# A two-layer MLP kernel: x times w_in by seven products on halves of a token tile, with weights streamed for every tile

## What is computed

```python
def _moe_ref(x, w_in, w_out, s, b):      # x (2304, 512), w_in (512, 2048), w_out (2048, 512)
    h = x @ w_in
    r = np.maximum(h, 0.0)
    g = s * (r * r) + b
    return g @ w_out

def _moe2_ref(x, w_in, w_out, alpha):
    h = x @ w_in
    g = np.maximum(h, 0.0) + alpha * np.minimum(h, 0.0)
    return g @ w_out

# reference: attention -> x; x = _moe_ref(x, ...); return _moe2_ref(x, ...)
```

## Time and profile before

| | us |
|---|---|
| median of 3 runs | 1132.96 (1132.89 to 1134.08) |
| the profiled execution, its own time | 1132.73 |
| its span in the trace | 1130.9 |
| TensorE busy | 1102.4 (97%) |
| VectorE busy | 524.1 (46%) |
| ScalarE busy | 518.0 (46%) |
| GpSimd busy | 263.9 (23%) |
| mean granted clock of TensorE | 0.998 |

### The profile page before, as it was taken

The page is one execution under the profiler, slowest core; times in us unless marked ns, Lnnn a source line. Parts: engine busy times, 40 slices in busy tenths (PEclk is TensorE's granted clock), DMA queues, the critical chain, the costliest instruction groups (busy, mean ns, idle before and its releaser), DMA issues.

```text
span 1130.9 us, 19159 instructions
## 1 busy us (share of the span) xinstructions
PE 1102.4 (97%) x5881; PEld 888.6 (79%) x5881; DVE 524.1 (46%) x1008; ACT 518.0 (46%) x925; POOL 263.9 (23%) x440
## 2 busy tenths in 40 slices
PE   6899999999999999999999999899999999999998
PEld 5677777777668888888888889788888888888887
DVE  6778888878833342242233236622332332232232
ACT  4677777777754432232232226633333333333343
POOL 2555565656554400000000007800000000000000
PEclk9999999999999999999999999999999999999999
DMA  6666565655311100000000004400000000000010
GB/s 154 149 165 145 135 150 129 151 131 128 92 34 52 47 19 0 0 0 0 0 0 0 0 0 131 131 1 1 27 11 0 0 37 0 0 37 0 0 39 19
DMA packets 100118, 59.75 MB, mean 53 GB/s; under 512 B 67040, under 2 KB 83440, under 8 KB 100080
## 3 DMA queue, kind: packets, MB, share of 16 engines
q1 hardware_dynamic: 100080, 59.28, 20.8%
HBM read 30.94 MB, written 4.72 MB: 32 GB/s over the span
## 4 chain that ended last, share of the span: by engine, by line
PE 89%; ACT 3%; POOL 3%; SPq 2%; issue 1%; DVE 1%; DMA 0%; ACTq 0%; DVEq 0%
PE psum L822 23%; PE psum L821 23%; PE psum L823 23%; PE psum L927 8%; PE psum L900 6%; PE psum L843 2%; ACT pt L566 2%; PE psum L845 2%; PE psum L829 2%; PE psum L897 1%; POOL wout_lo L471 1%; POOL win_lo L468 1%; SPq L366 1%; PE psum L908 1%; SPq L342 1%
## 5 line engine op out<-in xcount | busy, mean ns | idle before, releaser
L821 PE MATMUL psum<-x_hi,win_hi 128*128 128x512 f32 (+1 forms) x640 | 238.9, 373 | 1.4 <-DVE x_lo L752 1.4
L822 PE MATMUL psum<-x_lo,win_hi 128*128 128x512 f32 (+1 forms) x640 | 238.4, 373 | 0.0
L823 PE MATMUL psum<-x_hi,win_lo 128*128 128x512 f32 (+1 forms) x640 | 238.4, 372 | 0.0
L821 PEld LDWEIGHTS psum<-x_hi,win_hi 128*128 128x128 f32 x640 | 120.5, 188 | 25.2 <-DVE x_lo L752 2.5
L822 PEld LDWEIGHTS psum<-x_lo,win_hi 128*128 128x128 f32 x640 | 120.6, 188 | 23.0
L823 PEld LDWEIGHTS psum<-x_hi,win_lo 128*128 128x128 f32 x640 | 120.3, 188 | 23.2
L770 DVE SCALAR_TENSOR_TENSOR act_r<-act_n,nalpha,act_r 128x512 f32<-128x512 f32 (+1 forms) x80 | 55.8, 698 | 158.9 <-ACT act_r L624 158.6
L695 DVE TENSOR_REDUCE negm<-psum 128x1 f32<-128x576 f32 x144 | 108.0, 750 | 44.6 <-PE psum L845 41.5
L491 POOL TENSOR_SCALAR ex<-ex,none_in,rinv 128x576 f32<-128x576 f32 x144 | 118.8, 827 | 24.9 <-DVE rinv L714 23.2
L762 DVE SCALAR_TENSOR_TENSOR g_lo<-act_r,b_c,g_hi 128x512 fp32r<-128x512 f32 (+1 forms) x80 | 60.6, 758 | 134.3 <-ACT g_hi L616 134.3
L616 ACT ACTIVATE g_hi<-act_r,b_c 128x512 fp32r<-128x512 f32 (+1 forms) x80 | 54.6, 682 | 147.4 <-PE psum L823 124.8
(11 more groups left out here) (80 smaller groups left out, 1627.6 us busy)
## 6 DMA issues: line engine op xcount, KB each, us to landing
k_twice<-k_hi SPq DMA_DIRECT2D x64, 144.0 KB, 2.5
stage<-in_moe_w_out_dram SPq DMA_DIRECT2D x32, 256.0 KB, 2.7
k_low_half<-k_lo SPq DMA_DIRECT2D x32, 144.0 KB, 2.5
out_dram<-stage SPq DMA_DIRECT2D x18, 256.0 KB, 2.2
raw_q<-in_q_dram SPq DMA_DIRECT2D x32, 128.0 KB, 2.4
raw_k<-in_k_dram SPq DMA_DIRECT2D x32, 128.0 KB, 2.5
raw_v<-in_v_dram SPq DMA_DIRECT2D x32, 128.0 KB, 2.6
q_both<-q_hi SPq DMA_DIRECT2D x32, 128.0 KB, 2.3
```

What stands on the lines that cost most here:

```text
L821: nc.tensor.matmul(dst, lhs[0], rhs[0], start=first, stop=False)
L822: nc.tensor.matmul(dst, lhs[0], rhs[1], start=False, stop=False)
L823: return nc.tensor.matmul(dst, lhs[1], rhs[0], start=False, stop=final)
```

## The change

One pipeline of steps takes the place of the two layers' loops. A step is a pair of hidden chunks, j and j + 8 (`PJ` is 8), of one tile.

For a full tile w_in (two hidden chunks by four feature chunks) is taken as a 2 by 2 block matrix A, and x (four feature chunks by 512 tokens) as a 2 by 2 block matrix B of halves with two feature chunks and 256 tokens each. Instead of eight block products there are seven, in the scheme with 15 sums: four sums of w_in blocks (S1 to S4, `win_sum`), four of x blocks (T1 to T4, `x_sum`), and seven sums of products. One block product is 2 chunks by 3, so 6 matmuls of 256 columns, and a step has 42 of them where two chunks of before had 24 of 512. TensorE adds two products in PSUM where it can (`in_a` takes two, `in_c` and `in_d` two with a sum read between); the rest are `first_sum` on ACT (a copy of `in_a`) and `middle_sums` and `last_sums` on DVE (five additions of 256 columns, each of one PSUM and one SBUF operand). The rest tile of 256 tokens is computed with plain products.

TensorE's order in a step k is: `up_part1` (four products, 24 matmuls), `down` of step k-1 for its first hidden chunk (12 matmuls of 512), `up_part2` (three products, 18 matmuls, after `middle_sums` of step k), `down` of step k-1 for its second chunk.

Weights are no longer kept. Every step loads its 512 KB of w_in and 512 KB of w_out, for every tile anew, into two buffers each, and splits them: ACT casts 512, 256 and 1,024 columns of w_in and its sums and 1,024 of w_out, POOL makes the low parts of w_in and of one half of w_out (`w_low`, `wout_low`), DVE makes four weight sums (`w_sums`) and the low part of the other half. The x sums stand at j = 5 of the tile before, the casts and low parts of x at j = 7; ahead of a rest tile at j = 6. The finished tile is copied out of PSUM at j = 1 of the next (`acc_copy`).

The core of the diff:

```diff
+            def up_part1(layer, i, j):
+                par, k = j % 2, step_no(layer, i, j)
+                wait_alone(pe, r_ok, 2 * (k - 1))
+                pe.wait_ge(w_lo_ok, w_parts(layer, i, j) + FULL_W)
+                x_there(layer, i, j, 1)
+                product(in_a[par], par, A11, B11, True, False)
+                x_there(layer, i, j, 2)
+                product(in_d[par], par, S1, T1, False, True).then_inc(part1_a_done, 1)
+                x_there(layer, i, j, 3)
+                product(in_b[par], par, S2, T2, True, False)
+                product(in_c[par], par, S3, T3, False, True).then_inc(part1_done, 1)
+            def up_part2(layer, i, j):
+                par = j % 2
+                pe.wait_ge(mid_ok, full_no(layer, i, j) + 1)
+                x_there(layer, i, j, 4)
+                product(in_a[par], par, A12, B21, False, False)
+                x_there(layer, i, j, 5)
+                product(in_d[par], par, S4, B22, False, True).then_inc(part2_a_done, 1)
+                x_there(layer, i, j, 6)
+                product(in_c[par], par, A22, T4, False, True).then_inc(up_done, 1)
...
+            # VectorE, one step
+            def mlp_step(layer, i, j):
+                following = after(layer, i, j)
+                tile_after = after(layer, i, PJ - 1)
+                if j == 1 and tile_before(layer, i):
+                    acc_copy(*tile_before(layer, i))
+                if following and not is_rest(following[1]):
+                    w_sums(*following)
+                if not is_rest(i):
+                    middle_sums(layer, i, j)
+                wout_low(layer, i, j)
...
+                    if j == PJ - 3:
+                        x_sums(*tile_after[:2])
+                    if j == PJ - 1:
+                        x_low(*tile_after[:2], range(3))
+                if not is_rest(i):
+                    last_sums(layer, i, j)
+                for row in range(2):
+                    curve(layer, i, j, row)
+                for row in range(2):
+                    g_low(layer, i, j, row)
+                if j == PJ - 1 and not is_rest(i) and not is_rest(tile_after[1]):
+                    x_low(*tile_after[:2], range(3, FULL_X))
...
+            # GpSimd, one step
+            def mlp_step(layer, i, j):
+                following = after(layer, i, j)
+                if following:
+                    w_low(*following)
+                wout_low(layer, i, j)
...
+            # ScalarE, one step
+                if following:
+                    w_high(*following, range(2))
+                if not is_rest(i):
+                    first_sum(layer, i, j)
+                if following and not is_rest(following[1]):
+                    w_high(*following, [2])
+                wout_high(layer, i, j)
...
+                rectify(layer, i, j)
+                for row in range(2):
+                    g_high(layer, i, j, row)
```

More of the change, by code:

```diff
@@ new lines, in g_high @@
+            def g_high(layer, i, j, row):
+                par, k, n = j % 2, step_no(layer, i, j), width(i)
+                wait_alone(act, down_done, 2 * (k - 2) + row + 1)
+                act.wait_ge(t_ok, 2 * k + row + 1)
+                dst, src = g_hi[:, par, row, 0:n], act_r[:, par, row, 0:n]
+                if layer:
+                    nc.scalar.copy(dst, src).then_inc(g_hi_ok, 1)
+                else:
+                    nc.scalar.activation(dst, src, ACT.Identity, bias=b_c[:]).then_inc(g_hi_ok, 1)
@@ new lines, in acc_copy @@
+            def acc_copy(layer, i):
+                act.wait_ge(down_done, 2 * PJ * (layer * NT + i + 1))
+                if layer == 0:
+                    for c in range(CC):
+                        nc.scalar.copy(x_raw[:, c, bass.ds(i * TOK, width(i))], acc[c][:, 0:width(i)]).then_inc(acc_free, 1)
+                else:
+                    for sub in range(0, subs(i), 2):
+                        wait_alone(act, y_out[sub], DMA * i)
+                        nc.scalar.copy(y_sb[:, sub, :], acc[sub]).then_inc(y_ok[sub], 1)
@@ L965, in down1 @@
-            def down1(i, j, weight):
-                pe.wait_ge(g_ok, i * FC + j + 1)
-                wait(pe, w_ok, weight)
-                if j == 0:
-                    pe.wait_ge(acc_free, (i + 1) * DC)
-                for c in range(DC):
-                    lhs = [x[:, j, c * P:(c + 1) * P] for x in (wout_hi, wout_lo)]
-                    rhs = [x[:, j % 2, 0:width(i)] for x in (g_hi, g_lo)]
-                    mm = three(acc[c][:, 0:width(i)], lhs, rhs, j == 0, j == FC - 1)
-                mm.then_inc(down_done, 1)
@@ L1013 @@
+            mlp(pe, mlp_step)
+            for row in range(2):
+                down(1, FULL_TILES, PJ - 1, row)
 _INS = ["q", "k", "v", "tau", "moe_w_in", "moe_w_out", "moe_s", "moe_b", "moe2_w_in", "moe2_w_out", "moe2_alpha"]
```

693 lines of the change are left out of this document (403 added, 290 removed).

## The result

The changed kernel takes 1268.94 us (median; 1266.36 to 1271.02) where the kernel before takes 1132.93: 1.120 times, 95% interval 1.118 to 1.121. So it is 12.0% slower; the forecast was 9.7%, 1243 us, and the time lies inside the forecast's range of 1150 to 1290. The profiled execution took 1269.77 us, its span is 1268.0.

A forecast was written before the change was run, and what follows sets the result against it. DVE's path, with waits for POOL and ACT, was taken to bound full steps. 326.9 + 3 + 749 + 64 + 90 + 2 + 2 + 4 = 1241 us of span, so 1243 us, range 1150 to 1290.

The forecast's parts named there:

- TensorE's part: In full tiles, a step needs 10.44 us of matmuls, 0.64 less than before; 41 us over 64 steps.
- The engines' part: In full steps, DVE's path, shut out by POOL, sets 11.3 us in layer 1, 12.1 in layer 2: 749 us.
- the lock: In SBUF, DVE with two SBUF inputs and POOL exclude each other for a whole instruction; 2.6 us a step.
- the 0.20 us: At POOL's end, a shut-out DVE instruction starts 0.20 us before the rule's letter allows; the letter adds 38 us.
- Tile ends: At j = 5, 7 and 1, DVE's x sums, low parts and copies add in full: 64 us together.
- Rest tiles: In rest tiles, steps of 5.64 and 5.60 us, 90 us; POOL and DVE fit except x sums, 2 us.
- Start: Ahead of the MLPs, nine ACT casts add 4.97 us before the last products with v; MLPs start at 326.9.
- (a): In full steps and tile ends, the port costs half: layer 1 at 10.44, layer 2 at 11.2; 1154 us; chance 0.18.
- (b): In full steps, TensorE stays the bound at 10.44 us, tile ends cost 26 in all; 1124 us; chance 0.08.
- (c): At six tile ends, TensorE's clock falls after long waits, 9.5 us each, 57 in all: 1300 us; chance 0.10.
- (d): In TensorE's narrow matmuls, the weight load limits the pace at 0.19 us; excluded by starts 0.1175 apart, no chance given.

The follow-up runs named there:

- the split: POOL makes two low parts of 512 columns a full step, held until DVE reads PSUM, against DVE making all low parts, with later casts: 1162.77 us.
- the kernel with the other hand-over: DVE starts its sums after POOL's last normalisation, ACT makes three casts one position earlier, against the kernel with DVE's list reordered: 1149.80 us.
- undoing the hold: POOL's two waits on part1_done and part2_a_done removed, against the fastest: 1147.98 us.
- the fastest: ACT's u1 copy and w_out cast, DVE's 1,024-column low part and tile copy moved earlier at tile ends, against the kernel with the other hand-over: 1124.14 us.

## Why the prediction was right, and where its sizes were off

The path was the one forecast, and the sum was 27 us short: 2.8 at the start, 20.2 and 7.2 in the rest tiles, some 2 at the first step and the tail, less 5.0 in layer 2's full steps.

**TensorE's part: right in kind, 0.16 us a step short.** 10.44 us were summed, 10.60 is what a step takes once nothing else bounds it (POOL cut to one column, and all kernels after the split). The starts of its groups in such a stretch, with no wait between (timeline of PE, the kernel with the other hand-over):

```profile
911.68 0.28 PE L1153 MATMUL psum<-x_hi,w_hi 128*128 128x256 f32 x1
...
914.56 0.40 PE L1017 MATMUL psum<-wout_hi,g_hi 128*128 128x512 f32 x1
```

That is 2.88 us for 24 matmuls of 256 columns, 0.120 each and not 0.1175 as in the earlier trace rows; 42 × 0.0025 = 0.1 us of the difference; the rest is in the two groups of w_out. Seven products give 0.5 us a step against 11.08, some 31 us, not 41.

**The engines' part: right.** Steps of 11.33 and 12.12 us, at the very places where they were worked out; TensorE idle ahead of part 2, released by L902. Taking POOL's columns away removes the excess; undoing the hold brings 0.5 and 1.2 us a step back in a kernel with less than half of POOL's columns. The Trainium skill's rule ("SBUF — State Buffer", section "SBUF: two separate sides") has the lock; the 0.20 us that the forecast kept from the trace held again (`wout_lo` ends at 576.39; the rule's letter gives 576.53 there).

**Tile ends: right in sum.** The x sums cost +3.7 for 3.55, the last step +5.2 for 5.35, the copies +2.1 to 2.4 in layer 1 and +0.5 to 1.6 in layer 2 for 1.1. Against that, the last full tile is cheaper than counted: its last two steps make no or fewer weight sums for a rest tile (10.78 and 8.49 us for 12.1 in layer 2). I had left that out. That layer 1's full steps come to 392.94 for 392.9 is therefore in part luck: two errors of some 6 us cancel.

**Rest tiles: the term that was mis-sized.** "POOL's 3.9 us and DVE's 3.2 fit beside them, except for the x sums": 47 us were forecast for layer 1, 67.21 came. The step failed by its own rule: the lock was counted in full steps and forgotten here. DVE and POOL in a rest step:

```profile
745.61 2.56 POOL L528 TENSOR_TENSOR w_lo<-win_raw,w_hi 128x512 fp32r<-128x512 f32 x2 [4.40 <-ACT w_hi L605]
748.13 1.74 POOL L544 TENSOR_TENSOR wout_lo<-wout_raw,wout_hi 128x512 fp32r<-128x512 f32 x1
```

```profile
747.04 1.68 DVE L936 TENSOR_TENSOR wout_lo<-wout_raw,wout_hi 128x512 fp32r<-128x512 f32 x1 [1.50 <-ACT wout_hi L611]
748.64 1.78 DVE L865 TENSOR_TENSOR x_lo<-x_raw,x_hi 128x512 fp32r<-128x512 f32 x1
```

Both of DVE's stand ahead of the curve, and both are shut out, 1.0 and 1.1 us. Steps took 6.75 for 5.64, and those at the borders to full tiles 8.7 to 10.8, since a full tile's weights or `g` are made there. With POOL cut to one column this stretch takes 52.69 us, so some 14 of the 20 us are POOL's columns, and 6 are left at the borders. The last stretch of layer 2 is +7 for the forecast, and 5 of these go with POOL's columns (41.25 us for 46.62).

**Start: +2.8 for two reasons not in the sum.** The last products with v began 1.2 us later than summed (325.18 for 323.99) and took 1.5 us longer. ACT's casts cost 5 us, as counted. But DVE's early sums met POOL's last normalisations, for which the last copies of `pt` wait: two of them took 3.50 us together (0.83 each alone), and none took over 0.84 where the sums were held back. What this was worth by itself was not measured, since the casts moved in the same run. And the last products with v, after TensorE had waited 6.3 us, ran at the lower level for their first 3 us:

```profile
325.18 4.39 PE psum L1098 x20
```

against 2.91 in the earlier trace rows; the granted clock was 0.50 from 325.2 to 327 us, 0.54 to 328.3 and 1.00 behind that.

**Rivals.** (a) fell: DVE was shut out for 3.0 us a step by its records, and 2.6 were counted. (b) fell for this kernel; but what spoke for it, that "POOL and DVE need not meet if ACT feeds them at other moments", is what the last kernels use. That the fastest takes 1124.14 us, the very sum of (b), is in part luck: its steps are 10.60 us and not (b)'s 10.44, and those ahead of the rest tile are shorter than (b) had them. (c) came in part. The clock did fall at tile ends. TensorE had waited 1.9 us for `g_lo` (until 402.3) ahead of the first of these stretches, and 1.8 us for `g_lo` (until 428.8) and 3.75 for L902 (until 435.6) ahead of the second:

```profile
404.00:408.00 4.00, 3.58 (x13) 2.41 (x13) 3.14 (x7) 1.92 (x2) 1.71 (x3) 0.66 0.00 0
435.00:442.00 7.00, 6.37 (x26) 5.93 (x27) 5.03 (x8) 3.54 (x7) 4.09 (x2) 0.58 0.18 63
```

(stretch, busy PE, PEld, DVE, ACT, POOL, clock, DMA share, GB/s). The Trainium skill's rule that idle gaps bring the lower level back ("TensorE: Matmul & The Clock Gate", section "Why this matters for your kernels") agrees with these stretches. The 9.5 us a tile end were not paid: in layer 1 the last step and the two behind it (16.54 + 13.75 + 11.32 us) come within 1.3 us of the forecast without a fall (16.65 + 12.4 + 11.3). The likely reason, argued and not tested, is that a slower pace is taken out of TensorE's waits where it isn't the bound; at the start, where it was, it cost 1.5 us. (d) fell: the narrow matmuls start 0.120 us apart and not 0.19.

## What to carry to other kernels

When work is handed to GpSimd to relieve VectorE, look first at where VectorE's operands lie: beside instructions with both operands in SBUF, a part of GpSimd's time is added and not hidden (here 149 us for some 480 us of its work in the MLPs, and no chain showed it), and doing the work on VectorE alone can be faster; beside the sums that read PSUM it was free, and holding each of GpSimd's two instructions back by one semaphore was worth 24 us. Apply a rule found in one part of a program to its other parts too, the short tiles and the hand-overs, before the sum is closed. Work for the next tile belongs spread over the steps that have slack (11 us here), and in front of nothing that the matrix engine waits for.

## What the runs showed that I had not expected

- GpSimd's instruction with one tensor input (a normalisation of 576 columns, 0.83 us alone) is shut out by VectorE's sums in SBUF as well, up to 2.26 us. The earlier trace rows had shown it only beside a VectorE instruction with a PSUM operand.
- The length of the last wait does not decide alone whether the granted clock falls. In the changed kernel it was 0.50 from 404 to 406 us behind a single wait of 1.9 us, but 1.00 from 976 to 978 behind one of 2.7. In the fastest kernel, whose longest wait in the MLPs is 1.85 us, it stayed at 1.00 there, and its mean was 0.998.
- A pair of GpSimd instructions of 512 and 256 columns keeps VectorE out of both of two instructions in a row (1.53 and 0.97 us for 0.43): the engines alternate, one instruction each. VectorE's own length does not matter: an instruction of one column took 1.25 us in this way.
- Two seven-product kernels that compute the same differ by 13% (1268.94 and 1124.14 us) through who makes the low parts, and in which order.

What stays open: in the fastest kernel TensorE still waits 10.0 us for the third middle sum, in 14 places at tile ends. Whether these can be had by order alone, as the 25 us before them, was not tried.
